# Attention, routing, experts, dense: the last two half-steps of the attention loop written out behind a shorter loop

## What is computed

```python
def _attn_ref(r, k, v, w, u):
    state = np.zeros((B, H, D, D)); y = np.zeros_like(r)
    for t in range(S):
        kt, vt, rt, wt = (k[:, :, t], v[:, :, t], r[:, :, t], w[:, :, t])
        cur = np.einsum('bhd,bhe->bhde', u[None] * kt, vt)
        y[:, :, t] = np.einsum('bhd,bhde->bhe', rt, state + cur)
        state = wt[..., None] * state + np.einsum('bhd,bhe->bhde', kt, vt)
    return y
# x = y as 3072 rows of 384
# routed: e = argmax(x @ w_gate), scale = softmax(...)[e] * sigmoid(x @ w_output_gate)[e]
#         x = scale * (relu(x @ w1[e]) @ w2[e])                  8 experts, 384 -> 1024 -> 384
# dense:  out = relu(x @ w_in) ** 2 @ w_out                      384 -> 2048 -> 384
```

## Time and profile before

| | us |
|---|---|
| three runs | 927.06, 922.82, 923.64 |
| their median | 923.64 |
| the profiled execution | 920.35 |
| its span from first to last instruction | 918.5 |
| granted TensorE clock, mean of the span | 0.972 of full |

### The profile page before, as it was taken

The page is one execution under the profiler, slowest core; times in us unless marked ns, Lnnn a source line. Parts: engine busy times, 40 slices in busy tenths (PEclk is TensorE's granted clock), DMA queues, the critical chain, the costliest instruction groups (busy, mean ns, idle before and its releaser), DMA issues.

```text
span 918.5 us, 26421 instructions
## 1 busy us (share of the span) xinstructions
PE 882.4 (96%) x10836; PEld 812.9 (89%) x10837; DVE 486.6 (53%) x861; ACT 385.6 (42%) x701; POOL 158.5 (17%) x111
## 2 busy tenths in 40 slices
PE   4889999999999999999999999999999999999995
PEld 3789999998989999999999889889899899899895
DVE  5779999999753443244324490550550641631620
ACT  3567777777133343334323570440530530621610
POOL 1000000000264543354335201001001001001000
PEclk9999999999579999999999999999999999999998
DMA  7256666672064646565557501010010010000000
GB/s 290 80 215 245 240 242 242 243 266 63 27 219 143 156 128 125 180 157 134 120 177 191 91 2 59 9 34 26 9 43 17 9 43 26 0 9 27 1 15 20
DMA packets 45181, 99.20 MB, mean 108 GB/s; under 512 B 11904, under 2 KB 32032, under 8 KB 41184
## 3 DMA queue, kind: packets, MB, share of 16 engines
q1 hardware_dynamic: 40240, 86.02, 30.1%
q0 software_dynamic: 3936, 11.60, 4.5%
q10 hardware_dynamic: 976, 1.18, 0.4%
HBM read 83.84 MB, written 14.96 MB: 108 GB/s over the span
## 4 chain that ended last, share of the span: by engine, by line
PE 93%; DVE 3%; issue 2%; POOL 1%; ACT 1%; DMA 1%; POOLq 0%; DVEq 0%; ACTq 0%; SPq 0%
PE y_banks L1281 22%; PE h_banks L1271 22%; PE h_banks L1242 13%; PE y_banks L1255 12%; PE yt L320 5%; PE yt L342 4%; PE sc L262 3%; PE ms L354 3%; PE sc L257 2%; PE ms L282 2%; PE xt_ps L1223 1%; PE ms L294 1%; PE sc L260 1%; PE sc L269 1%; PE first_scale_ps L955 1%
## 5 line engine op out<-in xcount | busy, mean ns | idle before, releaser
L1281 PE MATMUL y_banks<-W,g 128*128 128x384 f32 x1152 | 200.8, 334 | 0.0
L1281 PEld LDWEIGHTS y_banks<-W,g 128*128 128x128 f32 x1152 | 200.0, 188 | 0.5
L1271 PE MATMUL h_banks<-yT,W 128*128 128x512 f32 x864 | 198.9, 392 | 0.8 <-POOL yT L1182 0.8
L1271 PEld LDWEIGHTS h_banks<-yT,W 128*128 128x128 f32 x864 | 162.1, 188 | 36.2 <-issue 1.2
L1346 ACT ACTIVATE relu<-h_banks 128x512 f32<-128x512 f32 x96 | 57.5, 599 | 235.0 <-PE h_banks L1271 228.5
L1242 PE MATMUL h_banks<-xT,W 128*128 128x448 f32 x576 | 119.7, 369 | 1.6 <-DVE xT L1370 1.6
L1255 PE MATMUL y_banks<-h,W 128*128 128x448 f32 x576 | 120.9, 368 | 0.0
L1242 PEld LDWEIGHTS h_banks<-xT,W 128*128 128x128 f32 x576 | 109.5, 190 | 10.4 <-issue 1.8
L1255 PEld LDWEIGHTS y_banks<-h,W 128*128 128x128 f32 x576 | 107.0, 188 | 8.6
L1423 DVE TENSOR_TENSOR relu<-relu 128x512 f32<-128x512 f32 x96 | 66.4, 692 | 66.0 <-ACT g L1350 66.0
L1441 DVE COPY stage<-y_banks 128x384 f32<-128x384 f32 x24 | 13.4, 558 | 163.9 <-PE y_banks L1281 163.9
(11 more groups left out here) (173 smaller groups left out, 1030.9 us busy)
## 6 DMA issues: line engine op xcount, KB each, us to landing
stage<-in_w SPq DMA_DIRECT2D x16, 1536.0 KB, 7.8
V<-in_vs SPq DMA_DIRECT2D x16, 1296.0 KB, 8.0
RK<-in_rkw SPq DMA_DIRECT2D x15, 1160.0 KB, 5.3
y_columns<-y_sb SPq DMA_DIRECT2D x8, 672.0 KB, 3.8
x_rows<-xs SPq DMA_DIRECT2D x32, 144.0 KB, 6.9
yb<-y_columns SPq DMA_DIRECT2D x5, 768.0 KB, 4.4
stage<-in_w_in SPq DMA_DIRECT2D x2, 1536.0 KB, 10.4
stage<-in_w_out SPq DMA_DIRECT2D x2, 1536.0 KB, 10.8
```

The source lines that it names most:

```text
L1271: ins = pe.matmul(h_ps[f % BANKS][:], w_in_of[wp][:, f // NF1, k, f % NF1 * P:(f % NF1 + 1) * P], yT[yp][:, k, :], start=(k == 0 and i == ...
L1281: ins = pe.matmul(y_ps[s % 2][:, 0:X], g[gp][:, f, s * P:(s + 1) * P], w_out_of[wp][:, f, :], start=(f == 0 and i == 0), stop=(f == NF2 - ...
```

## The change

`half_steps` loops seven times in place of eight, and then calls `body` for half-steps 16 and 17 as straight code, with the pair numbers known. `pair` answers None for a number of 16 or more, as it did for numbers below 0, and every helper leaves at once where its pair is None. So for half-step 16 the instructions of `x`, and for half-step 17 those of `x` and `y`, are not made. SP no longer stands in for the loads of pairs 16 and 17 except once (ACT's last pass through the loop still scales R of "pair 16", and waits for that), and waits for nothing of theirs before its last store. The order of what is left is as it was.

```diff
--- before.py
+++ after.py
@@ -94,14 +94,17 @@
 
     def pair(n, o):
 
-        if isinstance(n, int) and n * 2 + o < 0:
+        if isinstance(n, int) and not 0 <= n * 2 + o < N_PAIRS:
             return None
         return Pair(o % 2, n + o // 2, n * 2 + o)
 
     def half_steps(eng, body):
-        with eng.Fori(0, N_PAIRS // 2) as n:
+
+        with eng.Fori(0, N_PAIRS // 2 - 1) as n:
             for o in range(2, 4):
                 body(n, o)
+        for o in range(2, 4):
+            body(N_PAIRS // 2 - 1, o)
 
     def left(ap, s):
         return ap.rearrange("p (n two s) -> p n two s", two=2, s=s)[:, :, 0, :]
@@ -205,15 +208,12 @@
         last = N_PAIRS // 2 - 2
         for o in range(2, 4):
             rk_free(pair(last, o))
-            sp.sem_inc(rk_loaded[o % 2], 16)
+            if o == 2:
+                sp.sem_inc(rk_loaded[0], 16)
             load_half(sp, stage, o - 2, (w1, w2)[o - 2][0], staged)
             v_free(pair(last, o - 2))
             load_v(pair(last, o))
         store_x(pair(last, 1), last)
-        rk_free(pair(last, 4))
-        sp.sem_inc(rk_loaded[0], 16)
-        v_free(pair(last, 2))
-        sp.sem_inc(v_loaded[0], 32)
         store_x(pair(last, 3), last + 1)
 
     @block.gpsimd
@@ -488,7 +488,8 @@
 
             if p is None:
                 return
-            act.wait_ge(v_loaded[y.s], (y.twos + 1) * 32)
+            if y is not None:
+                act.wait_ge(v_loaded[y.s], (y.twos + 1) * 32)
             act.wait_ge(xt_full[p.s], p.twos + 1 + LEAD)
             if p.s == 0:
                 act.wait_ge(stored, p.twos * (4 * 16) + STORED_AHEAD)
```

## The result

| | before | changed |
|---|---|---|
| median of five runs, us | 923.64 | 935.9 |
| lowest to highest | 922.05 to 927.59 | 935.0 to 938.83 |
| profiled execution, and its span | 920.35, 918.5 | 935.0, 933.2 |

The ratio is 1.013, 95% interval 1.0106 to 1.0153: the change makes the kernel 12 us slower. The forecast was 927.0, with 921.0 to 932.0 as its range. It was wrong.

What follows compares the result with a forecast made beforehand. The prediction took each pair's chain of latencies to bound the last half-steps. Removal -0.9, stops +2.7 (half-step 16) and +0.8 (half-step 17), clock +0.8 gave +3.4: median 923.64 to 927.0 us, range 921.0 to 932.0.

Steps and rivals of the forecast that it cites:

- The bound: Last two half-steps: each pair's chain of latencies (11.3 us for pair 15) sets the time; phantom work stands beside it.
- The gain at DVE's third routing operation: End of attention: without phantom work DVE starts it at 223.05, not 223.72, a gain of 0.67 us.
- the mechanism of the loss: PE's new straight code arrives in pieces of about 64 matmuls, each asked for on entering the one before, 4.0 to 5.2 us.
- the two places in half-step 16: PE stops in `chunk_states` (0 to 1.3 us) and 4 matmuls into `scores(y,4)`; the latter puts +2.7 on the chain.
- the one in half-step 17: PE stops late in `within`, 16 matmuls into its last 48, delaying `from_states` by 0.8 us (0 to 1.0).
- the pieces were not there in time: Denies the rival that code pieces arrive in time, nothing stops and -0.9 is left: 922.7 us; chance 15%.
- the first piece was not missing: Denies the slower rival: code behind the loop asked for only at loop exit, +7.25, 930.9 us; chance 20%.
- the clock did not hold through routing: Denies the faster rival: earlier end of DVE's phantoms keeps the clock up in routing, 918 us; chance 5%.
- the time a piece takes under load: PE's straight code: a piece arrives 4.0 us after being asked for, or 5.2 under DMA load.
- The first stop: Half-step 16, about 10 matmuls into `chunk_states`: PE waits for the second piece, 0 to 1.3 us, taken as 0.5.
- the 14 and 12 named as signs: `turn_k` to last write would grow from 11.4 to about 14 us for pair 14, 11.3 to about 12 for pair 15.
- the clock: After the stop at `scores(y,4)` PE's clock may fall, slowing `from_states`: 1.7 us, half taken, +0.8; twice 1.7 if also half-step 17.

Runs made afterwards that it cites:

- the fourth experiment: Against the kernel before: DVE and ACT have straight code without phantom work, PE keeps its eight-pass loop and phantom matmuls; 925.17 against 924.83 us, ratio 1.0004.
- the second profile: Profile of the changed kernel run once more, unaltered, beside the kernel before on the same chip; 936.7 against 924.83 us, ratio 1.0133.

## Why the forecast was wrong

*Right.* The bound: the chain of pair 15 was not shortened by removing work; in the fourth experiment, without stops, it takes as long as before, and all that is gained is 0.68. The gain at DVE's third routing operation was forecast as 0.67 and is 0.62 to 0.68. Right too were the mechanism of the loss, the two places in half-step 16, and the one in half-step 17, which stands in the second profile. A piece is 128 records of PE; I had counted `turn_k`'s six matmuls as two records each, where they have one, so the edges stand 2 to 3 matmuls behind the forecast places. The rivals fell as the forecast thought likelier: the pieces were not there in time, the first piece was not missing (`scores(y,3)` and `turn_k` are on time, and in the changed kernel the instruction queue has no packet between 57.7 and 203.0), and the clock did not hold through routing.

*Wrong: the time a piece takes under load.* This is the step that failed. I took 4.0 to 5.2 us from the loop's first pass, where 5.2 stood beside a DMA share of 0.91, and put 4.6 in the sum. Measured from the end of one stop to the end of the next it is 6.13, 6.24 and 6.21 in half-step 16, with the share at 0.99 to 1.10 until the packet starts, and 3.81 with the engines idle. The higher end of my range was the nearest row, one case, and not an upper bound. Nor does the share tell the two places apart: over that row's own wait, 45.80 to 48.67, it was 1.02 too, and the packet started 2.9 us behind the entry, not 3.7 to 4.0. Why it is longer in half-step 16 stays open. The first stop became 2.3 to 2.6 for my 0.5, the second 3.1 to 4.1; together +6.2 on the chain and not +2.7. In the first profile the two pieces came 6.11 and 6.13 us after PE entered the one before (199.44, 205.55), where the forecast had 4.4 and 4.75, and PE entered the first 0.35 us later than assumed. That is the difference: `from_states` of pair 14 was forecast 7.9 behind its `turn_k` and stands 11.35 behind. From `turn_k` to the last write of a pair it is 19.3 and 13.7 us, for the 14 and 12 named as signs.

*Wrong: the clock.* I forecast a loss of at most 1.7 for one fall, since in the first pass it came back at once (0.89 and 0.69 in two windows), and put half of that in the sum. It fell in both profiles and stayed at 1.2 GHz for 13.6 us, through `from_states`, `turn_y` and, in the first, into half-step 17. There, in the first, it cost +1.6 and +2.4. The forecast saw the cost in `from_states`; from its start to that of `turn_y` it is only 0.3 longer (3.75 for 3.46), and `turn_y` alone lost 1.5. The row was read as the price of a fall; it was the price of one fall that ended early, with PE dense behind it. Here half a chain of waits stood behind it.

With 6.2 in place of 2.7, nothing for the stop in half-step 17, and 1.6 + 2.4 for the clock in place of 0.8, the same sum gives +9.3; the measure of the two half-steps is +9.55. The statement of the Trainium skill ("Runtime: NRT & Kernel Launch", "Instruction fetch mechanics") that crossing a block's edge is mostly hidden does not hold for this code: in half-step 16 of the changed kernel two edges out of two were not hidden. In half-step 17 of its first profile one was, at 1.2 GHz.

*Outside the two half-steps, and open.* The profiles put the rest of the 14.7 us between the spans as follows. The experts take 3.2 more in the changed kernel's first profile than in that of before, by the rate of a tile's matmuls, 15.04 or 14.76 us for 72 of them; of the eleven profiles five have 14.76 throughout, four 15.04, and two go from one to the other after the second tile. The changed kernel has both, so the edit does not decide it. The dense stage's first block takes 99.35 us in the profile before and 100.67 in the changed kernel's; five of the eleven profiles take 1.1 to 1.6 us more there, all of them among the seven without PE's phantom matmuls. Whether the change has a part in it no run says. And `turn_k` of pair 14 stands at 199.99 or 200.01 where PE keeps the loop of eight passes, and between 200.41 and 203.66 in the nine profiles where it does not, with stops of another size in the loop's first pass, although the code up to there is the same. I have no run that says why; together with the dense block it is of the size of the 2 to 3 us by which the difference in time, 12, exceeds the 9.5 of the measure.

## What to carry to other kernels

Work that runs beside the critical chain is free, and taking it out pays only where the chain's end waited for it, here 0.7 us. Straight code behind a hot loop is not free: ask how fast the engine will go through code that it has not run, find what such code cost at the loop's own first pass, and then ask what loads are in flight at the new place. Moving loads away helps only as far as the engine's own pace lets it. And a price read at one place is no upper bound at another, even where the DMA share reads the same.

## What the runs showed of the hardware that I had not expected

New code comes to PE in pieces of 128 records, some 64 of these fp32 matmuls. From the end of one stop to the end of the next it is 3.8 us with the DMA engines idle, and 6.1 to 6.2 in half-step 16 with bulk loads of SP in flight. The packet of 16 KB takes 0.96 to 1.37 us in the six cases of the table; what grows is the time before it starts, from 1.1 to 1.4 us to 3.7 to 4.0. Where the load is moved, the stop goes with it (3.86 us in half-step 17, where it had been 1.00). After the stops of half-step 16 the clock stayed at 1.2 GHz for 13.6 us in both profiles of the changed kernel; PE's busy share was 0.74 to 0.99 in the windows from 212 to 224 of the first, and 0.41, 0.91 and 0.73 in those of the second. In the two straight kernels with all matmuls kept it was 6.8 us. And fp32r matmuls of 448 columns run at one of two rates, 14.76 or 15.04 us for 72, which can differ between two runs of a kernel and within one.
